# Logits ahead of a wait, routing lists ahead of two fold turns, and two fold products moved across program ends, in an attention, experts and gated-layers kernel

## The reference, cut to what matters

```python
for t in range(S):                                   # attention, state per head
    cur = einsum('bhd,bhe->bhde', u[None] * kt, vt)
    y[:, :, t] = einsum('bhd,bhde->bhe', rt, state + cur)
    state = w * state + einsum('bhd,bhe->bhde', kt, vt)
do_compute = (x @ w_skip) > 0                        # experts
e_idx = argmax(x @ w_gate);  gate_w = softmax(x @ w_gate)[e_idx]
x = x + gate_w * (relu(x @ w1[e_idx]) @ w2[e_idx])   # where do_compute
a = x @ m_w1;  b = x @ m_w2                          # gated layers
out = ((a * b) @ m_w3) @ m_w_out
```

## Time and profile before

| | |
|---|---|
| time, median of 3 runs | 650.86 us (650.1 to 652.61) |
| the profiled execution: time, span | 651.47 us, 649.7 us |
| PE busy, share of the span | 614.7 us, 95% |
| DVE, ACT, POOL busy | 300.1, 217.1, 156.8 us |
| granted TensorE clock, mean | 0.98 |
| the four programs begin at about | 0, 138.9, 183.0 and 330.7 us |

### The profile page before, as it was taken

How to read it: one execution, slowest core, us unless ns; L and a number is a source line. 1 busy time by engine, 2 the same in 40 slices (tenths; PEclk the granted TensorE clock), 3 DMA queues, 4 the chain that set the end, 5 groups by cost and what they waited for, 6 DMA issues and landing times. The chain is left out here.

```text
span 649.7 us, 17457 instructions
## 1 busy us (share of the span) xinstructions
PE 614.7 (95%) x7374; PEld 548.8 (84%) x7374; DVE 300.1 (46%) x464; ACT 217.1 (33%) x382; POOL 156.8 (24%) x182
## 2 busy tenths in 40 slices
PE   7789898789999999999989999999999999999997
PEld 6688888646689999999968898888889888888886
DVE  5368887339157777887512132223224223223222
ACT  2144444222445554566313122123213123213212
POOL 6557776225324333234114000000000000000000
PEclk9779999799999999999999999999999999999999
DMA  9659999646137766555240003002003001001001
GB/s 134 113 119 189 186 178 207 195 153 228 33 133 265 258 251 224 184 214 209 84 140 27 0 1 98 0 1 98 0 1 97 1 1 49 1 1 48 1 0 49
DMA packets 104057, 67.77 MB, mean 104 GB/s; under 512 B 79458, under 2 KB 98052, under 8 KB 104016
## 3 DMA queue, kind: packets, MB, share of 16 engines
q1 hardware_dynamic: 75824, 57.88, 30.7%
q10 hardware_dynamic: 26144, 4.74, 4.3%
q0 software_dynamic: 2048, 4.58, 1.9%
HBM read 56.31 MB, written 12.58 MB: 106 GB/s over the span
## 5 line engine op out<-in xcount | busy, mean ns | idle before, releaser
L1440 DVE TENSOR_TENSOR gl_g_sb<-gl_a_sb,gl_pab 128x512 f32<-128x512 f32 x48 | 33.0, 687 | 186.4 <-ACT gl_a_sb L1417 186.4
L1360 PE MATMUL gl_pab<-gl_xT_hi,wm_lo 128*128 128x512 f32 x288 | 112.9, 392 | 0.0
L1360 PE MATMUL gl_pab<-gl_xT_lo,wm_hi 128*128 128x512 f32 x288 | 112.8, 392 | 0.0
L1360 PE MATMUL gl_pab<-gl_xT_hi,wm_hi 128*128 128x512 f32 x288 | 112.1, 389 | 0.0
L1417 ACT ACTIVATE gl_a_sb<-gl_pab 128x512 f32<-128x512 f32 x48 | 28.7, 599 | 183.9 <-PE gl_pab L1360 183.9
L1375 PE MATMUL gl_po<-gl_wf_hi,gl_g_hi 128*128 128x384 f32 x192 | 65.6, 342 | 0.7 <-DVE gl_g_lo L1442 0.7
L1375 PE MATMUL gl_po<-gl_wf_hi,gl_g_lo 128*128 128x384 f32 x192 | 64.7, 337 | 0.0
L1375 PE MATMUL gl_po<-gl_wf_lo,gl_g_hi 128*128 128x384 f32 x192 | 64.5, 336 | 0.0
L1360 PEld LDWEIGHTS gl_pab<-gl_xT_hi,wm_lo 128*128 128x128 f32 x288 | 54.0, 188 | 11.4
L1360 PEld LDWEIGHTS gl_pab<-gl_xT_lo,wm_hi 128*128 128x128 f32 x288 | 54.0, 188 | 10.5
L1360 PEld LDWEIGHTS gl_pab<-gl_xT_hi,wm_hi 128*128 128x128 f32 x288 | 54.1, 188 | 10.3
(11 more groups left out here) (197 smaller groups left out, 1147.3 us busy)
## 6 DMA issues: line engine op xcount, KB each, us to landing
ew_w_in<-in_moe_w SPq DMA_DIRECT2D x16, 1536.0 KB, 8.0
w_in<-in_moe_w SPq DMA_DIRECT2D x14, 512.0 KB, 7.2
k_in<-in_k SPq DMA_DIRECT2D x48, 96.0 KB
v_in<-in_v ACTq DMA_DIRECT2D x48, 96.0 KB
r_in<-in_r SPq DMA_DIRECT2D x48, 96.0 KB
xbuf<-x_nat SPq DMA_DIRECT2D x24, 192.0 KB
gl_x_in<-xbuf SPq DMA_DIRECT2D x12, 384.0 KB, 4.2
out<-gl_o_sb SPq DMA_DIRECT2D x12, 384.0 KB, 2.5
```

The lines of the kernel that those rows point to most:

```text
L1360: m = pe.matmul(p_ab[f % 2][w][:, :], a[:, w * KD + k, cols], b[t.slot][:, k, :], start=(k == 0 and n == 0), stop=(k == KD - 1 and n == 2))
L1440: dve.tensor_tensor(g_sb[f % 2][:, :], a_sb[f % 2][:, :], p_ab[f % 2][1][:, :], ALU.mult).then_inc(s_g, 1)
```

## The change

Four edits. In attention's loop the logits stand ahead of `inputs_ready` in PE's order, and `natural` has one more wait, for the count `s_Y` of the same tile. In its last steps product 0 is cut in another way: a quarter behind the transposes of x in step NT + 2 and three quarters behind the last logits, where two quarters stood behind `natural` in step NT + 1, one behind the transposes of x and one behind the last logits. In routing the list matmuls stand ahead of turn 6, product 5 and turn 7, and product 6 is gone from there. It stands in the experts' program, behind the last expert and ahead of the load of the overflow count, and ACT takes it there. In the gated layers product 7 is cut in half: quarters 0 and 1 at the start, 2 and 3 in the place of `keep_warm`.

```diff
             def natural(t):
+                wait(pe, s_Y, t.done())
                 wait(pe, s_YT, t.done())
...
-                if f is natural and at(c, j, NT + 1):
-                    fold.product(pe, 0, p_AU[:, 0, :], (0, 1))
                 if f is x_transposes and at(c, j, NT + 2):
-                    fold.product(pe, 0, p_AU[:, 0, :], (2,))
+                    fold.product(pe, 0, p_AU[:, 0, :], (0,))
                 if f is logits and at(c, j, NT + 3):
-                    fold.product(pe, 0, p_AU[:, 0, :], (3,))
-            schedule(pe, ((turns_ready, 0), (k_transposes, 0), (x_transposes, -3), (r_transposes, 0), (natural, -2), (inputs_ready, -1), (logits, -4),
+                    fold.product(pe, 0, p_AU[:, 0, :], (1, 2, 3))
+            schedule(pe, ((turns_ready, 0), (k_transposes, 0), (x_transposes, -3), (r_transposes, 0), (natural, -2), (logits, -4), (inputs_ready, -1),
...
                 fold.product(pe, 1, p_W[1], (2, 3))
-                for i in range(2, 7):
+                for i in range(2, 6):
                     fold.turn(pe, i, p_T[i % 2])
...
                 m.then_inc(s_list, 1)
+                fold.turn(pe, 6, p_T[0])
+                fold.product(pe, 5, p_W[1])
                 fold.turn(pe, 7, p_T[1])
-                fold.product(pe, 6, p_W[0])
...
-                for i in range(2, 7):
+                for i in range(2, 6):
                     fold.turned(act, i, p_T[i % 2])
...
+                fold.turned(act, 6, p_T[0])
+                fold.taken(act, 5, p_W[1])
                 fold.turned(act, 7, p_T[1])
-                fold.taken(act, 6, p_W[0])
...
                 rounds(pe, step, 2, E, 1, 0)
+                fold.product(pe, KF - 2, p_h[0][:, :, :].rearrange("p a b -> p (a b)"))
...
                 rounds(act, whole(act, (hidden_hi, 0), (w1_hi_, 1), (x_hi, 1), (wm_hi_, 0)), 2, E, 1, 0)
+                fold.taken(act, KF - 2, p_h[0][:, :, :].rearrange("p a b -> p (a b)"))
...
-                fold.product(pe, KF - 1, p_o[-1])
+                fold.product(pe, KF - 1, p_o[-2], (0, 1))
...
-                            keep_warm(pe, ident, p_o[0], 12)
+                            fold.product(pe, KF - 1, p_o[-2], (2, 3))
...
-                                fold.taken(act, f, p_o[-1])
+                                fold.taken(act, f, p_o[-2])
```

## The result

The changed kernel takes 645.28 us (median of 9 runs, 643.46 to 649.72), the kernel before beside it 651.65 us (9 runs, 650.1 to 655.36): ratio 0.992, 95% interval 0.989 to 0.995.

The account below looks back on a forecast made before the run. The prediction took SP's issuing to bound attention's loop, PE the routing, and scatter and x's load the experts' end. Loop 0, tail -0.1, routing -4.4 and seam +4.1 made -0.4, from 650.86 to 650.4 us; range 647.2 to 652.8.

Parts of the forecast that it names:

- The loop: Attention's loop: SP's unbroken issuing is the bound and PE's 5.5 us of stops are slack, so the edit gains 0.
- The anchor 122.90: End of attention's loop, where x_nat's last long idle ends: claimed to stay at 122.90, within 0.3 us.
- the prediction's own sign: Check at the end of attention's loop: the prediction is wrong if the 122.9 moves by more than 1 us.
- Rival 1: Attention's loop gives up its slack: 5.5 us more gain, 644.9 us; chance 12%.
- The tail of attention: Attention's last steps: same PE work with the wait at another place, -0.1 us, from -0.6 to +0.3.
- Lists ahead of two turns: Routing: product 6 leaves and the experts begin sooner, at 178.6, -4.4 us; bounds 2.4 and 4.57.
- Rival 2: Experts' first transposes: the gather is late, 652.5 us at the median landing, 654.9 at the latest; chance 8%.
- The seam: Experts' end to first gate matmul: x's load 2.7 us late, half of product 7 adds 1.4; +4.1 us.
- Rival 3: PE is put to half clock at the experts' end, losing 2.5 us: 652.9 us; chance 6%.
- rival 4: Experts' end: SP isn't held by ACT, x lands as before, +1.4 instead of +4.1, 647.7 us; chance 5%.
- The sum: Whole kernel: loop 0, attention's tail -0.1, routing -4.4, experts' end +4.1, together -0.4 us, so 650.4 us.

Follow-up runs that it names:

- act_loads: The kernel before, with the fold's four transfers (w3 twice, w_out in halves) issued by ACT in attention's last steps instead of by SP: 646.7 us, ratio 0.993.
- the change again: The whole change run once more beside the kernel before, for a second profile: 646.43 us, ratio 0.993.
- loop_only: The kernel before with only the loop's edit, logits ahead of the wait for states and the added wait: 648.48 us, ratio 0.995.
- peel_loop: The kernel before with PE's first round written out ahead of the loop, and the loop edit on top: 652.83 us, ratio 1.002.
- loop_act_loads: The kernel before with the loop edit alone and the fold's four transfers issued by ACT: 642.31 us, ratio 0.987.
- tail_only: The kernel before with only product 0 cut in another way in attention's last steps: 650.95 us, ratio 1.0005.
- fold_moves_only: The kernel before with only the lists ahead of two turns and products 6 and 7 moved: 650.44 us, ratio 0.998.

## Why the prediction was wrong

**The loop: the step that failed.** It is "what PE does sooner, SP doesn't issue sooner", and with it "With SP as the bound I take 0 ... The anchor 122.90 stays, within 0.3 us." That SP waits for nobody from 44 us on, at 17.1 us a round, was right and stayed right (85.53 to 102.56 in the changed kernel, 17.0); act_loads shows that what stands in SP's queue holds the anchor, by its data more than by its issues. What failed is the step from the run's length to its end. The earlier trace rows begin at 44 us; I didn't ask what releases the run's first issue at 40.45. SP had waited 12.3 us for PE's p_R until then, in the rounds where PE was late. There the loop edit brings SP forward, by 2.0 to 4.4 us against before: 39.7 to 40.6 in five kernels without the order and with SP's queue of the first round unchanged, 36.0 to 38.5 in five with it. The anchor moved with it, by 1.5, 2.8 and 4.6 us in the three with SP's transfers at their old place (the change, the change again, loop_only), and from tile 8's load to the anchor it took 81.6 to 83.4 us with the order and 82.2 to 83.3 without. By the prediction's own sign, an anchor that moves by more than 1 us, it was wrong. loop_only measured 3.1 us for the term that I had at 0.

**Rival 1 gave the time, not for its reason.** 644.9 was its figure, 645.28 was measured. That was luck: the 5.5 us of stops in the earlier trace rows were not what was won. Most of them came back ahead of k_dec, and with the transfers out of SP's queue they are worth 0.7 to 1.2 us by the profiles. "Find the gaps of the busiest engine", the rule of the Trainium skill ("Perfetto Trace Analysis", Optimization Strategy) that I had beside this rival, would have named the right edit for gaps that hardly paid. The other reading of the Trainium skill (the same page, "What DMA-bound means"), an issuing queue without gaps, fits the rounds, where SP waits for nobody, though the busy DMA engines there are a rival; at the anchor it is not borne out: the stores were issued only 1.2 us sooner, and the anchor came 3.7 us sooner.

**Why PE is sooner there** is settled in part. Shown: the added wait alone doesn't do it; and the mean granted clock of all runs is higher with the order in each of five pairs of kernels (0.988 for 0.981 in loop_only, 0.980 for 0.974 in peel_loop). In loop_only PE runs the last steps of its first pass at 2.4 GHz instead of 1.2, and its work there takes 18.1 us instead of 21.8. But act_loads and loop_act_loads differ in the stops (9.2 us and 6.1 in the pass) and not in the work (19.5 and 19.7), and the change again gained 2 us at tile 8's load with 0.50 from 28 to 36. So clock and stops share the gain differently from profile to profile, and how the order acts on either stays open. Filling the wait with other work doesn't do it.

**The tail of attention**, -0.1: right, 1.0005. What I didn't see is that its length varies with the clock from execution to execution, 17.44 us in the profile after with 0.50 from 120 to 132, 15.45 in the change again. In the five kernels with SP's run shortened it is 14.3 to 15.1, in loop_only and tail_only 15.0.

**Lists ahead of two turns**, -4.4: right. Measured 44.09 to 39.66, 4.43, and by the reason given: gathers at 173.95 and 175.48 for 173.9 and 175.4, transposes at 178.50. Rival 2, the late gather, did not happen.

**The seam**, +4.1: right in kind, 3.4 to 3.9 measured. SP left the barrier 6.9 us behind the last expert matmul (6.7 forecast): ACT reached the barrier 1.3 to 1.4 us behind the begin of its copy, where I took 1.2. Counted from the begin of the last expert matmul, x's load was issued 2.8 to 2.9 us later than before (2.7 forecast), the transposes followed 4.44 and 3.99 us behind it (4.46 before), and the half product in the place of the filler turns put the gates 1.05 us later behind the transposes (1.4 forecast). Rival 3 did not happen: granted clock 1.00 from 329 to 337.3. Nor did rival 4: x waited for ACT.

**The sum.** Routing and seam together, -0.3 in my sum, are -0.6 and -1.1 in the two profiles after, and fold_moves_only is 1.2 us faster by its runs. With the 3.1 of the loop edit and nothing of the tail that makes 4.3, where the two measurements of the change give 5.1 and 4.4 by their ratios. The experts' stage varies from 142.9 to 146.9 us even among the eleven profiles of kernels without the fold's moves (mean 145.0); the five with them have 142.8 to 144.3 (mean 143.8). Whether the moves shorten it by some 1.2 us, as theory B of fold_moves_only had it, or this is scatter, stays open.

## What to carry to other kernels

A queue that issues without waits can set the length of a stretch, but not its begin: ask what released its first issue, and treat the stretch before it as one more stage with its own bound. An engine's first pass over a loop's code has other limits (stops for code, granted clock) than the rounds that the groups by line average over; look at it on its own timeline. When what stands in a queue is the bound, look at which transfers could go to another queue, or to another time: four transfers moved to ACT, and to later steps, were worth about as much as the whole change. Then see whether it was their issuing or their data that stood in the way: here mostly the data.

## What the runs showed of the hardware

PE's first pass over the loop's code had four to six stops without a releaser, 0.2 to 3.6 us each and some 5 us apart, with six packets on an instruction queue up to 44 us (before) and none from 44 to 100. With the first round written out ahead of the loop (peel) there were ten packets, stops in both rounds, and a kernel 4 us slower by its ratio. In the first pass of the kernel before the granted clock was 0.50 from 28 to 40 us. With full DMA engines (share 1.05, 334 GB/s from 113 to 122 us in the kernel before) a store's wait ended some 8 us behind its issue, where a round earlier it was 2.3. DMA issued in SP's waits wasn't free: 2.5 MB more in the first round came with a start of SP's run over 2 us later (42.79 for 40.45).
